# Expert outputs added to the result by accumulating indirect DMAs, with one loop over stretches and three widths of the first product

## What is computed

```
noisy = x @ w_gate + log1p(exp(x @ w_noise)) * noise        # x: 2304 x 512, 8 experts
top2, weights = two best experts of each row, softmax of their two values
for each row and each of its two experts e:
    out[row] += weight * (relu(x[row] @ w1[e]) @ w2[e])      # w1[e]: 512 x 1024, w2[e]: 1024 x 512
```

## Time and profile before

| | us |
|---|---|
| median of 3 runs | 1189.87 (1185.16 to 1189.94) |
| profiled execution | 1201.1 |
| its span, first to last instruction | 1199.4 |
| mean granted TensorE clock | 0.96 |
| PE busy | 1088.4 (91%) |
| DVE busy | 514.0 (43%) |
| POOL busy | 511.5 (43%) |
| ACT busy | 374.3 (31%) |
| DMA packets | 156.08 MB, mean 130 GB/s |

### The profile page before, as it was taken

The page is one execution under the profiler, slowest core; times in us unless marked ns, Lnnn a source line. Parts: engine busy times, 40 slices in busy tenths (PEclk is TensorE's granted clock), DMA queues, the critical chain, the costliest instruction groups (busy, mean ns, idle before and its releaser), DMA issues. The chain is left out here.

```text
span 1199.4 us, 18749 instructions
## 1 busy us (share of the span) xinstructions
PE 1088.4 (91%) x6340; PEld 989.3 (82%) x6341; DVE 514.0 (43%) x1142; ACT 374.3 (31%) x903; POOL 511.5 (43%) x289
## 2 busy tenths in 40 slices
PE   4999999989999999999993899999999999995770
PEld 4888888867899899999992789898989898984660
DVE  5887778765322333425144422222222232236126
ACT  3777777755222221313131412121212020210100
POOL 7776777720000202012011455555555566657205
PEclk9999999999999999999996799999999999997795
DMA  8644444417599401011011734343443333324218
GB/s 230 146 100 100 98 98 98 98 46 217 194 378 392 170 0 52 5 47 44 9 52 53 269 111 161 130 166 129 149 140 131 140 131 140 131 88 120 81 51 308
DMA packets 83988, 156.08 MB, mean 130 GB/s; under 512 B 9329, under 2 KB 26993, under 8 KB 83953
## 3 DMA queue, kind: packets, MB, share of 16 engines
q1 hardware_dynamic: 70576, 107.40, 29.0%
q0 software_dynamic: 13376, 48.24, 12.0%
HBM read 91.66 MB, written 63.96 MB: 130 GB/s over the span
## 5 line engine op out<-in xcount | busy, mean ns | idle before, releaser
L1396 PE MATMUL ps_hT<-xT_high,ew_high 128*128 128x384 f32 (+1 forms) x512 | 161.5, 315 | 18.4 <-DVE hT_low L1480 14.0
L784 POOL DMA_INDIRECT expert_rows<-x_rows,slot_idx x36 | 37.8, 1049 | 305.9 <-DVE slot_idx L919 296.7
L1396 PE MATMUL ps_hT<-xT_high,ew_low 128*128 128x384 f32 (+1 forms) x512 | 160.2, 313 | 2.2 <-issue 2.2
L1396 PE MATMUL ps_hT<-xT_low,ew_high 128*128 128x384 f32 (+1 forms) x512 | 160.2, 313 | 2.2 <-issue 2.1
L1480 DVE SCALAR_TENSOR_TENSOR hT_low<-ps_hT,hT_high 128x384 fp32r<-128x384 f32 (+1 forms) x128 | 62.3, 490 | 171.1 <-ACT hT_high L1445 153.9
L1411 PE MATMUL ps_y<-ew_high,hT_high 128*128 128x512 f32 x320 | 128.9, 403 | 0.0
L1411 PE MATMUL ps_y<-ew_high,hT_low 128*128 128x512 f32 x320 | 125.6, 392 | 0.0
L1411 PE MATMUL ps_y<-ew_low,hT_high 128*128 128x512 f32 x320 | 124.6, 389 | 0.0
L1396 PEld LDWEIGHTS ps_hT<-xT_high,ew_high 128*128 128x128 f32 x512 | 99.2, 194 | 20.9 <-DVE hT_low L1480 14.2
L1445 ACT ACTIVATE hT_high<-ps_hT 128x384 fp32r<-128x384 f32 (+1 forms) x128 | 55.7, 437 | 193.9 <-PE ps_hT L1396 180.6
L1490 DVE COPY y_tile<-ps_y 128x512 f32<-128x512 f32 x40 | 27.7, 692 | 176.5 <-PE ps_y L1411 176.5
(11 more groups left out here) (213 smaller groups left out, 2725.2 us busy)
## 6 DMA issues: line engine op xcount, KB each, us to landing
spare<-e_w POOLq DMA_DIRECT2D x14, 1024.0 KB, 5.9
w_raw<-e_w POOLq DMA_DIRECT2D x14, 1024.0 KB, 5.5
ex_rows<-expert_rows SPq DMA_DIRECT2D x45, 256.0 KB, 3.9
q_raw<-qT SPq DMA_DIRECT2D x36, 288.0 KB, 4.2
k_raw<-kT SPq DMA_DIRECT2D x36, 288.0 KB, 5.5
expert_rows<-w_raw SPq DMA_DIRECT2D x8, 1280.0 KB, 14.6
expert_out_early<-w_raw SPq DMA_DIRECT2D x8, 1280.0 KB, 14.7
expert_out<-y_tile SPq DMA_DIRECT2D x40, 256.0 KB, 2.3
```

Of the source, the lines that this page charges most:

```text
L784: nc.gpsimd.indirect_dma_start(out=rows_dram, out_offset=bass.IndirectOffsetOnAxis(ap=slot_idx[:, k, t:t + 1], axis=0), in_=x_rows[:, t, : ...
L1396: mm = nc.tensor.matmul(ps_hT[q % HS][:, 0:rows.stop - rows.start], lhsT[:, c, f * P:(f + 1) * P], rhs[:, c, rows], start=(n == 0), stop=( ...
```

## The change

The experts' results are no longer stored and gathered; each scaled tile is added to `out` in DRAM by an indirect DMA that accumulates. Both `place_outputs` and `order_weights`, the two output buffers, both sets of gathers, the mixing and the 18 stores at the end are gone. In their place:

- Each row that routing sends carries four more numbers (2064 bytes instead of 2048): the token, both weights and the first choice's number. So the five small DVE operations of f == 7 (den, reciprocal, second weight, two copies) come before the slots in f == 6; the two copies of the slots are dropped.
- SP zeroes `out` (9 DMAs of up to 0.5 MB) instead of the unused stretches.
- `plan_experts` gives, for each stretch: first row, expert, rows left, and which of the widths 576, 608 and 640 holds its rows.
- All engines run the first stretch, one loop over the middle ones, and the last stretch. In the middle ones PE loads the width's number and runs one of three bodies of the second half of the first product (320, 352 or 384 columns). Here that is 576, 576, 608, 608, 576 and 608 rows for the second to seventh stretch. The last stretch turns no further rows.
- SP issues the weight loads that POOL issued, for each stretch, behind the load of the next rows.
- DVE finds, in each stretch after the fifth unit of the first product, the output row and the weight of each of the 640 rows (`know_rows`). This waits until all additions of the stretch before have landed. The copy out of PSUM multiplies by the weight; there are five `y_tile` buffers.
- POOL issues one accumulating DMA for each tile, between its cuts of the weights.

Cut to its core:

```diff
@@ route, f == 6 @@
+                    dve.wait_ge(e2_ready, g + 1)
+                    link(nc.vector.tensor_scalar(t1["den"][:], t1["e2"][:], 1.0, 1e-9, ALU.add, ALU.add), base)
+                    link(nc.vector.reciprocal(x_rows[:, :, M + 1], t1["den"][:]), base)
+                    link(nc.vector.tensor_tensor(x_rows[:, :, M + 2], t1["e2"][:], x_rows[:, :, M + 1], ALU.mult), base)
+                    link(nc.vector.tensor_copy(x_rows[:, :, M], consts[:, bass.ds(C["token"] + g * TT, TT)]), base)
+                    link(nc.vector.tensor_copy(x_rows[:, :, M + 3], t1["idx1"][:]), base)
...
-                        link(nc.vector.tensor_copy(slots[:, k, bass.ds(g * TT, TT)], t1[slot][:]), base)
@@ experts, gpsimd @@
+            def add_y(g, j):
+                pool.wait_ge(y_taken, TILES * g + j + 1)
+                pool.sem_inc(waited, 1)
+                nc.gpsimd.indirect_dma_start(out=out, out_offset=bass.IndirectOffsetOnAxis(ap=out_rows[:, j:j + 1], axis=0),
+                                             in_=y_tile[j][:], in_offset=None, compute_op=ALU.add).then_inc(y_added[j], 16)
+
+            def stretch(g, before, last):
+                if before is not None:
+                    pool.wait_ge(y_done, TILES * g)
+                    for k in range(PIECES, 2 * PIECES):
+                        cut_high(g, k)
+                        cut_low(before, k)
+                if last:
+                    for j in range(TILES):
+                        add_y(g, j)
+                    return
+                pool.wait_ge(h_done, UNITS * (g + 1))
+                cut_high(g + 1, 0)
+                cut_low(g, 0)
+                add_y(g, 0)
+                cut_high(g + 1, 1)
+                add_y(g, 1)
+                cut_low(g, 1)
+                for j in range(2, TILES):
+                    add_y(g, j)
@@ experts, sync @@
+            def next_x(g):
                 sp.wait_ge(x_turned, TILES * g + TILES)
...
+                sp.wait_ge(rows_known, 2 * (g + 1))
+                load_x(g + 1)
...
+            with sp.Fori(1, last_but_one) as g:
+                next_x(g)
+                next_second(g, g - 1)
+                next_first(g)
@@ experts, tensor @@
+                if before is None or last:
+                    first_product(g, before, 1)
+                else:
+                    step = pe.value_load(widths_i[0:1, bass.ds(g, 1)], min_val=0, max_val=len(WIDTHS) - 1)
+                    for k, width in enumerate(WIDTHS):
+                        with pe.If(step == k):
+                            first_product(g, before, 1, width)
@@ experts, vector @@
+            def know_rows(g, first):
+
+                for j in range(TILES):
+                    dve.wait_ge(x_loaded[j], 16 * (g + 1))
+                    if not first:
+                        dve.wait_ge(y_added[j], 16 * g)
+                left, key = rows_left[:, bass.ds(g, 1)], expert_key[:, bass.ds(g, 1)]
+                place = consts[:, C["place"]:C["place"] + TILES]
+                nc.vector.tensor_scalar(is_held[:], place, left, None, ALU.is_lt).then_inc(rows_read, 1)
+                nc.vector.tensor_scalar(is_first[:], x_rows[:, :, M + 3], key, None, ALU.is_equal).then_inc(rows_read, 1)
+                nc.vector.tensor_copy(token_of[:], x_rows[:, :, M]).then_inc(rows_read, 1)
+                nc.vector.tensor_copy(out_rows[:], nowhere[:]).then_inc(rows_read, 1)
+                nc.vector.tensor_copy(weight_of[:], x_rows[:, :, M + 2]).then_inc(rows_read, 1)
+                dve.wait_ge(rows_read, READS * (g + 1))
+                dve.sem_inc(waited, 1)
+                nc.vector.copy_predicated(out_rows[:], is_held[:], token_of[:]).then_inc(rows_known, 1)
+                nc.vector.copy_predicated(weight_of[:], is_first[:], x_rows[:, :, M + 1]).then_inc(rows_known, 1)
...
-                nc.vector.tensor_copy(y_tile[s][:], ps_y[s][:]).then_inc(y_taken, 1)
...
+                nc.vector.tensor_scalar(y_tile[j][:], ps_y[j % YS][:], weight_of[:, j:j + 1], None, ALU.mult).then_inc(y_taken, 1)
+
+            def stretch(g, before, last):
                 for q in range(UNITS):
                     low_h(g, q)
+                    if q == FC // 2:
+                        know_rows(g, before is None)
```

More of the change, by code:

```diff
@@ L665, in gated_product_and_routing @@
     w1_high, w1_low, w2_high, w2_low, wo_high, wo_low = parts
-    rows_dram, outs_dram, slots, weights, counts = store
+    rows_dram, out, counts = store
     DC, N = xT.shape[1], xT.shape[2]
@@ L1105, in plan_experts @@
[L1105 to L1111 removed]
+    link(nc.vector.tensor_tensor(each(E, K), along(held, K), across(limits, E), ALU.is_gt))
@@ new lines, in plan_experts @@
+    link(nc.vector.tensor_reduce(stretches, each(E, K), AX.X, ALU.add))
+    link(nc.vector.tensor_scalar(stretches, stretches, 1.0, None, ALU.max))
+    link(nc.vector.tensor_tensor(each(E + 1, E), earlier, across(stretches, E + 1), ALU.mult))
+    link(nc.vector.tensor_reduce(bounds, each(E + 1, E), AX.X, ALU.add))
+    for k in range(ends_i.shape[1]):
+        link(nc.vector.tensor_scalar(ends_i[:, k:k + 1], bounds[:, E:E + 1], -float(k), None, ALU.add))
+    add_up(number, bounds[:, 1:E], ones, ALU.is_ge, expert_of)
@@ L1371, in _ @@
-            sp.wait_ge(out_stored, 16 * T)
+            second = expert(1)
+            sp.wait_ge(first_low, COLUMNS)
+            for k in range(PIECES):
+                load_w(second, k)
+            for k in range(PIECES):
+                sp.wait_ge(second_low, k + 1)
+                load_w(second, PIECES + k)
+            total, _, last_but_one, last_but_two = stretches(sp)
+            next_x(0)
+            next_first(0)
+            with sp.Fori(1, last_but_one) as g:
+                next_x(g)
+                next_second(g, g - 1)
+                next_first(g)
@@ L1445, in high_h, with stretch @@
                 nc.scalar.activation(hT_high[:, f, rows], ps_hT[q % HS][:, 0:rows.stop - rows.start], ACT.Relu).then_inc(hhigh, 1)
+            def stretch(g, before, last):
+                for q in range(UNITS):
+                    high_h(g, q)
+                if not last:
+                    for j in range(TILES):
+                        high_x(g + 1, j)
             for loaded in ahead_loaded:
@@ L1457, in _ @@
                 nc.scalar.copy(high, loaded).then_inc(second_high, 1)
-            with act.Fori(0, bound(act, E, E)) as g:
-                for q in range(UNITS):
-                    high_h(g, q)
-                for j in range(TILES):
-                    high_x(g + 1, j)
+            through(act, stretch)
         @block.vector
```

393 lines of the change are left out of this document (145 added, 248 removed).

## The result

The changed kernel takes 1210.15 us in the median (1205.7 to 1211.28), the kernel before, timed beside it, 1189.9: a ratio of 1.0171, interval 1.0133 to 1.0209. It is slower by some 20 us, where I forecast 1176.6 and a range of 1125 to 1200.

What follows compares the result with a forecast made beforehand. PE was taken to set the pace in steady stretches. Gains of 74.0 us, less 0.8 for routing, 48.0 for the `know_rows` stall and 11.9 for clock, left 13.3: 1189.9 to 1176.6 us, range 1125 to 1200.

Steps and rivals of the forecast that it cites:

- comes back to 57.8 us, 29.3 gained: Last stretch: without `place_outputs`, slow matmuls and early gathers it falls from 87.1 to 57.8 us, 29.3 gained.
- the main cost: `know_rows` on DVE, held by POOL's cuts of W2, stalls PE at unit ten: 48.0 us over seven stretches.
- The clock: Slow matmuls after each PE stall: 1.7 us lost a stretch, 11.9 in seven.
- The widths: Narrower first-product units in six middle stretches: 5.4 ns a column and unit, 12.4 us gained.
- nothing, under PE: Routing: sixteen bytes more in a row and the other zeroing cost nothing, hidden under PE.
- Earlier groups hide it behind PE's products: Routing: five small operations before the slots cost only 0.8 us, in the last group; PE's products hide the rest.
- I take 0: PE's value loads, branches and jumps in six stretches: cost taken as 0, within 0 to 24 us.
- I take 3.5: Tail: the last accumulating DMA lands in 3.5 us, bounds 2.3 and 7; tail 6.0 instead of 36.5 us.
- rival 3: PE from unit ten in seven stretches: the clock stays slow, 49 us lost instead of 11.9; 1214 us, chance 0.13.
- Rivals 1 and 2: `know_rows` reads slip past POOL's cuts, 1133.2 us, chance 0.23; no PE stall at all, 1116.7 us, chance 0.05.
- Rival 4: Jumps starve PE behind the chosen body, before the second product: 6 x 2.0 = 12 us, 1188.6, chance 0.05.
- rival 5: All stretches take the full width, through wrong counts or body: 12.4 us less gained, 1189.0, chance 0.04.

Runs made afterwards that it cites:

- experiments 7: Kernel before with 32 bytes put ahead of the turned x and nothing of the change: 1193.43 us, ratio 1.0046.
- experiment 12: Kernel before, unchanged, profiled in a second execution (also called the second execution): 1187.02 us, ratio 0.9991, span 1184.7.
- the late `know_rows` alone: Changed kernel with `know_rows` behind the fourteenth unit of the first product instead of the fifth: 1152.04 us, ratio 0.9669.
- experiment 9: Changed kernel with `know_rows` behind the fourteenth unit, five routing operations back at f == 5, 96 bytes padding behind gathered rows: 1132.72 us, ratio 0.9544.

## Why the prediction was wrong

Against the second execution the sum missed by 37.9 us, 24.6 + 13.3; against the medians by 33.6, 20.3 + 13.3. Each row of the table above has its step, known to the 3 us or so by which executions of one program differ.

- **Last stretch, 14.5 us: "comes back to 57.8 us, 29.3 gained".** The largest miss. It was read from a span 11.2 us above the median, and of the three profiled executions (this one and those of experiments 7 and 12) the nine issue gaps and the slow matmuls around them stood in that one alone. Against the execution shown this row is -22.3, near the forecast; it is the other times of the kernel that it misses. The kernel had 73.25 - 57.26 = 16.0 us to give there, of which 14.2 are the stall and the rest the clock behind it. The prediction saw the risk ("some of the last stretch's loss may be missing in them") and put it into its range, but took the full 29.3 off the median. With 16.0 the same sum would have been a gain of nothing.
- **Middle stretches, 10.9 us: "the main cost".** By the experiments the six changed as follows: gaps +37.7, clock +13.7, place of the buffers +7.6, widths -10.1; sum 48.9. The stall was right to 0.4 us a stretch (6.7 forecast; 6.3). The clock was 2.3 us a gap where I took 1.7, within the bounds (whose upper end the prediction gives as 7.1 and works out as 7.0). The widths gave 10.1 of 12.4. The place of the buffers stood nowhere in the prediction: it says of the sixteen bytes more in a row that they cost "nothing, under PE", and they move every buffer behind them. PE covers the writing of a longer row, but not the place of its own operands: that term was put at nothing without a reason.
- **Routing, 6.6 us: "Earlier groups hide it behind PE's products".** They don't. The slots release a scatter, the scatter's landing releases ACT's copy, and the copy PE's turning; the five operations lengthened that chain in every group. PE stood 5.3 us for it in four groups; how the rest of the 6.6 divides between the last group and the difference of executions stays open. I had named the engine that covers the step, not the margin.
- **First stretch, 3.1 us: "I take 0"** for value loads and branches. PE stands 1.9 us for four value loads between the turnings and the first product, and without them the stretch was 3.0 shorter; the place of the buffers gives 1.8 (69.41 us with the late `know_rows` alone, 67.58 in experiment 9). The 1.4 us of stall that I forecast did not come: the seven operations ran behind POOL's subtractions, in 0.16 to 0.22 us each.
- **Tail, 2.8 us: "I take 3.5"** for the landing. From the end of the issue to the end of the span it is 1209.3 - 1204.1 = 5.2, within my bounds; and the issue, costed at 0.95 by rows 8, is 1.56 for one that adds. The dearer issue was listed among the signs of being wrong, and the slower landing stood in the range.

Of the rivals, rival 3 gave 1214, close to the time, by a mechanism that was not it: the clock took 2.3 us a stretch, not 7.0, and below the 3.6 from which it was to decide. Rivals 1 and 2 fall, since copy_predicated was held and the fourth cut decided. Rival 4 had one gap of 1.1 us, not six of 2.0; rival 5 falls with the widths measured. That the change is a loss rests on the stall: without it, 1152. And what it can give is 1131.6, 4.7% below the kernel before.

## What to carry to other kernels

- Small operations put on the critical engine's feeder are not small when they share ports with long ones elsewhere: look at what runs beside the new place for as long as they may be held, and move them, or the long ones, to where they do not meet. Either order was worth some 58 us here.
- Before a gain is read off one profiled execution, set its span against the median. If it lies above, what is irregular in it (gaps that no wait explains) may not be there to win.
- A longer row or a new buffer moves those behind it. Here PE was fast only with its operands, streamed or loaded, on multiples of 128 bytes; put them there, and compare the distance of like matmuls before and after.

## What the runs showed of the hardware that I had not expected

- PE's pace depends on where its SBUF operands start. Output tiles (24 matmuls of 512 columns and a turning) are 5.94 or 5.95 us apart in the median with buffers on multiples of 128 bytes, 6.02 at 64 past, 6.03 to 6.05 at 32 past; the step from 128 to 32 is shown in both kernels. With no turning, 24 matmuls take 5.49 against 5.63 us. The Trainium skill, SBUF — State Buffer, section Operand start alignment, asks for a multiple of the element size and says that this is about legality, not speed. Both kinds of operand count: displaced was the streamed one in the first product and the loaded one in the second. Units of 256 columns took 1.36 against 1.44 us and those of 320 the same, 1.76. Why stays open, and no run had the operands on another multiple of 128.
- An indirect DMA that adds costs POOL 1.56 us to issue, one that only writes 0.97, and from the end of the last issue to the end of the span it is 5.2 us against 3.6.
- After gaps of 6.2 to 6.4 us the matmuls lost 1.8 to 3.0 us to the clock, at 0.5 in the records; after one of 14.2 us 1.8. The loss did not grow with the gap, and why it differs between gaps of one length stays open.
- One execution of the kernel before stood 8.3 us on PE's own issue beside 18 gathers, another not at all, with the same program (experiment 12). What made the difference stays open.
